# Attention scores as three fp32r products of high and low parts, with both heads' last queries in one block

## What is computed

```python
    scores = scale * np.matmul(q, k.transpose(0, 1, 3, 2))      # scale = 1/8
    scores = np.where(block_i >= block_j, scores, -1000000000.0)  # blocks of 64 positions
    scores = scores - np.max(scores, axis=-1, keepdims=True)
    attn = np.exp(scores)
    attn = attn / (np.sum(attn, axis=-1, keepdims=True) + 1e-09)
    return np.matmul(attn, v).astype(np.float32)
    ...
    h = x @ w_in
    g = np.maximum(h, 0.0) + np.log1p(np.exp(-np.abs(h)))
    return (g @ w_out).astype(np.float32)
```

## Time and profile before

| | us |
|---|---|
| median of three runs | 718.02 |
| lowest, highest | 717.34, 724.31 |
| the profiled execution | 717.23 |
| its span | 715.5 |
| TensorE busy in the span | 680.9 (95%) |
| VectorE, ScalarE, GpSimd busy | 435.8, 404.2, 161.5 |

### The profile page before, as it was taken

The page is one execution under the profiler, slowest core; times in us unless marked ns, Lnnn a source line. Parts: engine busy times, 40 slices in busy tenths (PEclk is TensorE's granted clock), DMA queues, the critical chain, the costliest instruction groups (busy, mean ns, idle before and its releaser), DMA issues.

```text
span 715.5 us, 12988 instructions
## 1 busy us (share of the span) xinstructions
PE 680.9 (95%) x4006; PEld 524.7 (73%) x4006; DVE 435.8 (61%) x1047; ACT 404.2 (56%) x991; POOL 161.5 (23%) x224
## 2 busy tenths in 40 slices
PE   6999999999979999999999999999999999999594
PEld 5565656565568999898888898899889988754342
DVE  5676767676636576667657765776577657824122
ACT  3676667676755566656655666556656655531110
POOL 2867676767620000001000100100020001002011
PEclk9999999999999999999999999999999999999798
DMA  8555755553220000200010011002000100296600
GB/s 192 122 154 134 197 136 156 135 154 103 68 86 1 2 0 1 90 1 10 23 65 1 7 44 44 0 0 66 21 9 3 44 0 3 97 381 197 222 23 17
DMA packets 79616, 53.88 MB, mean 75 GB/s; under 512 B 61208, under 2 KB 64280, under 8 KB 79568
## 3 DMA queue, kind: packets, MB, share of 16 engines
q1 hardware_dynamic: 75872, 50.47, 23.8%
q10 hardware_dynamic: 1920, 1.48, 0.7%
q0 software_dynamic: 1776, 1.33, 0.7%
HBM read 41.31 MB, written 16.28 MB: 80 GB/s over the span
## 4 chain that ended last, share of the span: by engine, by line
PE 62%; DVE 4%; issue 2%; DMA 1%; ACT 1%; ACTq 0%; DVEq 0%; POOL 0%; POOLq 0%
PE hidden L903 9%; PE rows_out L916 9%; PE hidden L905 9%; PE hidden L904 9%; PE rows_out L914 9%; PE rows_out L915 9%; PE hidden L1009 4%; PE rows_out L1023 3%; DMA other_x<-x_sorted 1%; PE turned_y L941 1%; DVE log L1308 1%; DVE g L1309 1%; PE rows_out L1018 1%; PE misc L950 1%; DVE series L1305 1%
## 5 line engine op out<-in xcount | busy, mean ns | idle before, releaser
L903 PE MATMUL hidden<-x_parts,w_in_high 128*128 (+1 forms) x384 | 132.7, 345 | 3.1 <-DVEq L1311 2.9
L1123 ACT ACTIVATE mag<-hidden 128x384 f32<-128x384 f32 x96 | 47.1, 491 | 151.3 <-PE hidden L905 151.1
L905 PE MATMUL hidden<-x_parts,w_in_low 128*128 (+1 forms) x384 | 129.6, 337 | 0.0
L904 PE MATMUL hidden<-x_parts,w_in_high 128*128 (+1 forms) x384 | 129.5, 337 | 0.0
L856 POOL DMA_INDIRECT x_sorted<-y,slot x18 | 20.4, 1136 | 416.6 <-DVE slot L1360 412.9
L916 PE MATMUL rows_out<-w_out_high,g_low 128*128 128x512 f32 x288 | 114.1, 396 | 0.0
L914 PE MATMUL rows_out<-w_out_high,g_high 128*128 128x512 f32 x288 | 113.7, 395 | 0.4 <-DVE g_low L1318 0.4
L915 PE MATMUL rows_out<-w_out_low,g_high 128*128 128x512 f32 x288 | 113.5, 394 | 0.0
L903 PEld LDWEIGHTS hidden<-x_parts,w_in_high 128*128 128x128 f32 x384 | 72.2, 188 | 11.0 <-DVEq L1311 4.1
L444 ACT ACTIVATE probs<-scores,neg_max 128x128 f32<-128x128 f32 (+3 forms) x128 | 67.0, 529 | 20.3 <-DVE neg_max L520 16.5
L266 POOL TENSOR_SCALAR probs<-probs,inverse 128x128 f32<-128x128 f32 (+3 forms) x128 | 65.6, 532 | 51.9 <-DVE inverse L541 51.9
(11 more groups left out here) (169 smaller groups left out, 1065.4 us busy)
## 6 DMA issues: line engine op xcount, KB each, us to landing
whole_w<-in_moe_w_dram SPq DMA_DIRECT2D x12, 1024.0 KB, 10.6
x_heads<-x_pair SPq DMA_DIRECT2D x16, 288.0 KB, 2.1
x_raw<-x_heads SPq DMA_DIRECT2D x6, 768.0 KB, 5.5
out_dram<-y SPq DMA_DIRECT2D x6, 768.0 KB, 4.0
q_nat<-in_q_dram SPq DMA_DIRECT2D x32, 128.0 KB, 2.6
v_nat<-in_v_dram SPq DMA_DIRECT2D x32, 128.0 KB, 2.4
stage<-in_moe_w_in_dram SPq DMA_DIRECT2D x8, 512.0 KB, 3.8
stage<-in_moe_w_out_dram SPq DMA_DIRECT2D x8, 512.0 KB, 4.0
```

The source lines that it names most:

```text
L903: nc.tensor.matmul(o, win["high"][:, k, cols], high, start=(k == 0), stop=False)
L904: nc.tensor.matmul(o, win["high"][:, k, cols], low, start=False, stop=False)
L905: last = nc.tensor.matmul(o, win["low"][:, k, cols], high, start=False, stop=(k == K - 1))
```

## The change

Queries and keys are each kept as a high part, rounded to fp32r, and a low part, the remainder. `qT` becomes `qT["high"]` and `qT["low"]`, `kT` the same. The scores are high x high + high x low + low x high, all in fp32r, which is one pass of the array per product. ScalarE writes the high parts of the full chunks (`round_qk`, two new instructions a step: q between the copies p2a and p2b, k behind the copy p3a), and VectorE writes the low parts in the place of its copies, waiting for ScalarE's. For the ends VectorE does both parts, in six instructions in the place of two.

For block 4 the last 64 queries of both heads stand side by side in `q_last`, 128 columns wide, with zeros where the other head's dimensions are. So one matmul over the whole array serves both heads: six of 288 columns in the place of four (eight records) of 288 columns on quarters. The block's result has the same layout.

For room, q and the tails of q, k and v are loaded into parts of `probsT` that hold no probabilities; the DMAs keep their number, sizes and waits, apart from the addresses.

```diff
+        qT = {h: sb(own, f"qT_{h}", [P, 2, FULL * P], F32R) for h in ("high", "low")}
+        kT = {h: sb(own, f"kT_{h}", [P, 2, S], F32R) for h in ("high", "low")}
+        q_last = {h: sb(own, f"q_last_{h}", [P, 2, P], F32R) for h in ("high", "low")}
...
+        PRODUCTS = (("high", "high"), ("high", "low"), ("low", "high"))
...
                 if i < FULL:
-                    for two in range(2):
-                        d = slice(two * D, two * D + D)
-                        last = nc.tensor.matmul(tile[:, two, :], qT[d, p % 2, P * i:P * i + P],
-                                                kT[d, p % 2, 0:P * (i + 1)], start=True, stop=True)
+                    for a, b in PRODUCTS:
+                        for two in range(2):
+                            d = slice(two * D, two * D + D)
+                            last = nc.tensor.matmul(tile[:, two, :], qT[a][d, p % 2, P * i:P * i + P],
+                                                    kT[b][d, p % 2, 0:P * (i + 1)],
+                                                    start=(a, b) == PRODUCTS[0], stop=(a, b) == PRODUCTS[-1])
                 else:
-                    for n in range(4):
-                        two, half = n % 2, (n // 2 + n) % 2
-                        d = slice(two * D, two * D + D)
-                        last = nc.tensor.matmul(tile[d, half, :], qT[d, p % 2, P * i:S],
-                                                kT[d, p % 2, half * (S // 2):(half + 1) * (S // 2)], start=True, stop=True)
+                    for half in range(2):
+                        for a, b in PRODUCTS:
+                            last = nc.tensor.matmul(tile[:, half, :], q_last[a][:, p % 2, :],
+                                                    kT[b][:, p % 2, half * (S // 2):(half + 1) * (S // 2)],
+                                                    start=(a, b) == PRODUCTS[0], stop=(a, b) == PRODUCTS[-1])
...
+            def round_qk(p, name):
+                at, b = p - 1, p % 2
+                act.wait_ge(s["turned_ready"], turned_count(at, name))
+                if name == "q":
+                    ins = nc.scalar.activation(qT["high"][:, b, 0:P * FULL], bank(at, "q"), ACT.Copy, scale=SCALE)
+                else:
+                    ins = nc.scalar.copy(kT["high"][:, b, 0:P * FULL], bank(at, "k"))
+                ins.then_inc(s["qk_high"], 1)
...
                 if turn:
                     copy_probs(p - 1, "p2a", 2, (0,))
+                if load:
+                    round_qk(p + 1, "q")
+                if turn:
                     copy_probs(p - 1, "p2b", 2, (1,))
...
                 if turn:
                     copy_probs(p - 1, "p3a", 3, (0,))
+                if load:
+                    round_qk(p + 1, "k")
...
                 if name == "q":
-                    ins = nc.vector.tensor_scalar(qT[:, b, 0:P * FULL], bank(at, "q"), SCALE, None, ALU.mult)
+                    dve.wait_ge(s["qk_high"], 2 * p + 1)
+                    ins = nc.vector.scalar_tensor_tensor(qT["low"][:, b, 0:P * FULL], bank(at, "q"), SCALE,
+                                                         qT["high"][:, b, 0:P * FULL], ALU.mult, ALU.subtract)
                 elif name == "k":
-                    ins = nc.vector.tensor_copy(kT[:, b, 0:P * FULL], bank(at, "k"))
+                    dve.wait_ge(s["qk_high"], 2 * p + 2)
+                    ins = nc.vector.tensor_tensor(kT["low"][:, b, 0:P * FULL], bank(at, "k"),
+                                                  kT["high"][:, b, 0:P * FULL], ALU.subtract)
                 else:
-                    nc.vector.tensor_scalar(qT[:, b, P * FULL:S], bank(at, "ends")[:, 0:TAIL], SCALE, None, ALU.mult)
-                    ins = nc.vector.tensor_copy(kT[:, b, P * FULL:S], bank(at, "ends")[:, TAIL:2 * TAIL])
+                    last = slice(P * FULL, S)
+                    q_end, k_end = bank(at, "ends")[:, 0:TAIL], bank(at, "ends")[:, TAIL:2 * TAIL]
+                    own_part = [slice(two * D, two * D + D) for two in range(2)]
+                    for d in own_part:
+                        nc.vector.tensor_scalar(q_last["high"][d, b, d], q_end[d, :], SCALE, None, ALU.mult)\
+                            .then_inc(s["ends_high"], 1)
+                    nc.vector.tensor_copy(kT["high"][:, b, last], k_end).then_inc(s["ends_high"], 1)
+                    for two, d in enumerate(own_part):
+                        dve.wait_ge(s["ends_high"], 3 * p + two + 1)
+                        nc.vector.scalar_tensor_tensor(q_last["low"][d, b, d], q_end[d, :], SCALE, q_last["high"][d, b, d],
+                                                       ALU.mult, ALU.subtract)
+                    dve.wait_ge(s["ends_high"], 3 * p + 3)
+                    ins = nc.vector.tensor_tensor(kT["low"][:, b, last], k_end, kT["high"][:, b, last], ALU.subtract)
                 ins.then_inc(s["copied_by_vector"], 1)
```

More of the change, by code:

```diff
@@ L129, in attention, with v_chunk @@
         probsT = sb(own, "probsT", [P, 2, CH, S])
+        k_nat = sb(own, "k_nat", [P, 2, FULL, 2, D])
+        q_full = [probsT[:, b, FULL, 0:FULL * P].rearrange("p (c a d) -> p c a d", c=FULL, a=2) for b in range(2)]
+        k_full = [k_nat[:, b, :, :, :] for b in range(2)]
+        q_end, k_end, v_end = ([probsT[:, b, c, 0:P].rearrange("p (a d) -> p a d", a=2) for b in range(2)] for c in (1, 2, 3))
+        def v_chunk(p, two, c):
+            return v_nat[:, p % 2, two, c, :] if c < FULL else v_end[p % 2][:, two, :]
         neg_max = sb(own, "neg_max", [P, CH, 2])
@@ L191, in load_qk @@
                     sp.wait_ge(s["turned_ready"], turned_count(p - 3, "ends"))
-                for nat, src, loaded in ((q_nat, qf, q_loaded), (k_nat, kf, k_loaded)) if p > 0 else ((q_nat, qf, q_loaded),):
+                for full, end, src, loaded in ((q_full, q_end, qf, q_loaded), (k_full, k_end, kf, k_loaded))[:2 if p > 0 else 1]:
                     for two in range(2):
-                        sp.dma_start(nat[:, p % 2, 0:FULL, two, :],
+                        sp.dma_start(full[p % 2][:, :, two, :],
                                      src[2 * p + two, 0:FULL * P, :].rearrange("(c p) d -> p c d", p=P))\
                           .then_inc(loaded[p % 2], 16)
-                    sp.dma_start(nat[0:TAIL, p % 2, FULL, :, :],
+                    sp.dma_start(end[p % 2][0:TAIL, :, :],
                                  src[2 * p:2 * p + 2, FULL * P:S, :].rearrange("a p d -> p a d")).then_inc(ends_loaded[p % 2], 16)
@@ L310, in turn_qk @@
                 if name == "ends":
-                    for n, nat in enumerate((q_nat, k_nat)):
+                    for n, end in enumerate((q_end, k_end)):
                         last = nc.tensor.transpose(to[:, n * TAIL:(n + 1) * TAIL],
-                                                   nat[0:TAIL, p % 2, FULL, :, :].rearrange("p a d -> p (a d)"),
+                                                   end[p % 2][0:TAIL, :, :].rearrange("p a d -> p (a d)"),
                                                    ident[0:TAIL, 0:TAIL])
                 else:
-                    nat = q_nat if name == "q" else k_nat
+                    full = q_full if name == "q" else k_full
                     for c in range(FULL):
                         last = nc.tensor.transpose(to[:, c * P:(c + 1) * P],
-                                                   nat[:, p % 2, c, :, :].rearrange("p a d -> p (a d)"), ident[:])
+                                                   full[p % 2][:, c, :, :].rearrange("p a d -> p (a d)"), ident[:])
                 last.then_inc(s["turned_ready"], 1)
@@ L362, in mix_left @@
                     for two in range(2):
-                        last = nc.tensor.matmul(mixed[two * D:two * D + D, 0, P * c:SPLIT], v_nat[:, p % 2, two, c, :],
+                        last = nc.tensor.matmul(mixed[two * D:two * D + D, 0, P * c:SPLIT], v_chunk(p, two, c),
                                                 probsT[:, two, c, P * c:SPLIT], start=(c == 0), stop=(c == 1))
@@ L375, in mix_right @@
                         last = nc.tensor.matmul(mixed[two * D:two * D + D, 1, lo - SPLIT:S - SPLIT],
-                                                v_nat[:, p % 2, two, c, :],
+                                                v_chunk(p, two, c),
                                                 probsT[:, two, c, lo:S], start=(c == 0), stop=(c == CH - 1))
@@ L473, in copy_right @@
                 nc.scalar.copy(x_pair[:, SPLIT:S], mixed[:, 1, 0:S - SPLIT]).then_inc(s["mixed_right_copied"], 1)
+            for name in ("q", "k"):
+                round_qk(0, name)
             for p in range(PAIRS + 2):
-                now, turn = p < PAIRS, 0 < p <= PAIRS
+                now, turn, load = p < PAIRS, 0 < p <= PAIRS, p < PAIRS - 1
                 if p > 1:
@@ L507, in _ @@
             step = Chain(dve, s["sums_step"])
-            nc.vector.memset(v_nat[TAIL:P, :, :, FULL, :], 0.0)
+            for b in range(2):
```

(4 more changed lines are left out.)

16 lines of the change are left out of this document (6 added, 10 removed).

## The result

| | before | after |
|---|---|---|
| median of the timed runs, us | 717.87 (4 runs) | 733.89 (4 runs) |
| lowest, highest | 717.34, 724.31 | 729.79, 737.29 |
| ratio, 95% interval | | 1.0204 [1.0161, 1.0247] |
| the profiled execution, its span | 717.23, 715.5 | 735.79, 734.0 |
| first scores | 8.56 | 9.96 |

Both intervals lie clear of 1 and hold 2%, so the loss is sure and that it is more than 2% is not. The forecast was 722.6 us, with a range of 711.5 to 729.

A forecast was written before the change was run, and what follows sets the result against it. Two balanced loops of about 11.92 us, TensorE's and one through VectorE and GpSimd, were taken to bound the kernel; +4.2 (14 steps), +0.9 (start) and -0.5 (last step) made +4.6, so 722.6 us, range 711.5 to 729.

The forecast's parts named there:

- six at 0.13: VectorE's `ends` copies: six instructions for two at a pitch of 0.13 us, +0.52 us in the loop; step +0.30.
- the stage's end: Last step of the attention stage: loads nothing and keeps the gain of blocks 2 to 4, -0.5 us.
- First scores: Start of the attention stage: first scores move from 8.56 to about 9.70 us, +1.1, or +0.9 after block 3's gain.
- The second loop: Copy of p3b, `ends`, inverse, GpSimd's scalings, p1: sets the changed step at about 12.22 us; chance 0.57.
- p1 waits for GpSimd: Sign of being right: TensorE idles before p1 on GpSimd's scaling, which follows 0.30 us later.
- `ends` for k's low part: Sign of being right: TensorE's `ends` transposes wait for VectorE's low part of k, a stall of 0.32 us.
- The costs of the products: TensorE's score groups: 0.73 us for block 2, 0.90 for block 3; TensorE's work falls by 0.46 to 11.46 per step.
- serialized heads: Rival: the two heads' fp32r products do not run side by side; TensorE's step 13.5 us, total 742; chance 0.10.
- loads that show: Rival: weight loads add 0.4 us in blocks 2 and 3, step 12.6, total 728; chance 0.10, shared with slow short products.
- The rival of GpSimd's port: VectorE's subtractions wait behind GpSimd's split, low q until 107.6; +1.5 us a step, total 743; chance 0.08.
- The rival that TensorE stays the bound: Attention step 11.46 to 11.78 us if the second loop has slack or `ends` is cheaper; 712.0 with 11.46; chance 0.15.
- 0.15 us a step either way: Uncertainty of the likeliest case's step, which with the start gave its own range of 718.5 to 727 us.

The follow-up runs named there:

- e3: Kernel after, with `ends` as four whole-width instructions, second head's last queries not put apart (scores wrong): step 11.88 us against 12.60; 711.25 us, not comparable.
- e11: Kernel after, each of the two half-partition `ends` instructions for q's high part cut in two of 32 columns: step 12.75 us, 740.43 us (one run).
- e6: Kernel after with 19 useless matmuls filling TensorE's gaps at the start and in step 0: 735.56 us, 1.0140 of the kernel before.
- e10: Kernel after, unchanged, measured a second time: 736.18 us, 1.0235 of the kernel before.
- e2: Kernel before with VectorE's early inverse moved ahead of its copy of k: 721.61 us, 1.0029 of the kernel before.
- e12: Kernel after with inverse moved, DMA-built block, filled gaps, k sooner and feed-forward's first load one step later: 714.85 us, 0.9943 of the kernel before.
- e1: Kernel after with VectorE's early inverse moved ahead of its copy of k: 722.28 us, 1.0072 of the kernel before.
- e5: Kernel after with inverse first and q's last queries laid block-diagonally by two DMAs, `ends` four whole-width instructions: 728.00 us, 1.0027 of the kernel before.

## Why the prediction was wrong

The mechanism was right and the sign of its sum too; the size was not, and a second effect was missing.

**The step that failed: "six at 0.13".** The loop, from rows of both kernels:

| part of the loop, us | before | forecast | after |
|---|---|---|---|
| p1 to the copy of p3b | 8.89 | 8.67 | 8.59 |
| copy of p3b to the first of `ends` | 0.61 | 0.61 | 0.61 |
| `ends`, to the inverse | 0.26 | 0.78 | 1.23 |
| inverse to GpSimd | 0.49 | 0.49 | 0.49 |
| GpSimd to p1 | 1.67 | 1.67 | 1.68 |
| step | 11.92 | 12.22 | 12.60 |

The pitch of 0.13 us was read from neighbours of the same 128 partitions and charged for instructions that go from one half to the other and to the whole. Four of the six pitches cross a change of first partition, and there the next instruction waits for the whole length of the one before, 0.22 to 0.26 us instead of 0.13, 0.96 in all instead of 0.52: that is nearly the whole 0.45 us that was missing (e3, e11). The rule of the Trainium skill cited under e11 could have been applied before; with the length of 0.21 us in the earlier trace rows for the four held ones it would have given an estimate of 4 x 0.21 + 2 x 0.13 = 1.10 us for `ends` instead of 0.78, and a step of 12.54. Against it the high part of k came 0.08 us sooner than reckoned. So a step costs +0.68, not +0.30: over 14 steps 9.5 us in the place of 4.2. The pattern of the calculation also stopped one place too early: p1 of the last step waits as well (its `ends` were made in step 14), so the stage's end gave nothing back, +0.38 instead of -0.5.

**What was missing: the clock at the start.** First scores came at 9.96 instead of 9.70, again by the pitch: `ends` takes 1.24 us there too. That TensorE's gaps there grow to 1.15 and 1.44 us, and that the granted clock then falls to 1.2 GHz for 17 us, was in no term: 2.9 us (e6 against e10). That those gaps are the whole cause is not shown (e2, above).

By the profiled attention stage: forecast +4.6, found +13.9. The steps explain 5.3 of the 9.3 us between, the clock 2.9, and the last step and the start's pitch 1.1. Between the forecast 722.6 and the median 733.9 lie 11.3 us, so 2 more stay open. The pitch alone would have made 728, still in the range; it took the clock as well to leave it.

**What held.** The second loop, invisible in TensorE's busy share, sets the step; p1 waits for GpSimd and `ends` for k's low part. The costs of the products held to 0.01 us, those of 64 rows included: heads side by side, no weight load visible in groups of 384 and 512 columns. The rivals of serialized heads and of loads that show fell; the row tells against the sentence in "TensorE: Matmul & The Clock Gate" of the Trainium skill (Part 3, The mechanism) that a weight load overlaps only a matmul in other rows, as it did in the stream of full-array products. The rival of GpSimd's port fell too: q's low part took 0.69 us at 115.44, inside GpSimd's split of 114.39 to 116.76, and not 1.21 as in the earlier trace rows. What "SBUF — State Buffer" of the Trainium skill (Who interferes with whom) says of an operation with at most one SBUF input, that it does not contend, agrees with this row. The rival that TensorE stays the bound was false for this kernel, but its price was nearly right: with the second loop shortened (e12) the same products run in 11.60.

**The range.** It ended at 729 because the bounds that were worked out were nearly all on TensorE's side. The deciding loop had 0.15 us a step either way, from no row, and its new term, six times 0.13, a single value and no upper bound, although no row showed an instruction on one half of the partitions next to one on the other.

## What to carry to other kernels

- Two loops in balance share one busy row. Before costing an edit, find the waits whose sum is small but whose count is about that of the steps, add up that loop from rows, and charge the edit to each loop by itself.
- A pitch between instructions is a fact about that pair of neighbours, their first partitions included. Where the loop that decides gets a new kind of neighbour, that term needs its upper bound first; and it pays to let the DMA lay data out so that the engine works on whole width.
- Look at the granted clock wherever an edit lengthens a wait of TensorE at the start, and try the cheap order changes (a small instruction ahead of a long one) before judging a change by its time. Here one such move gave back most of the loss (e1), and with the layout by the DMA, the filled gaps, k sooner and the later load +2% became -0.6% (e12).

## What the runs showed of the hardware

- VectorE: neighbours of 32 or 64 columns that begin at the same partition start 0.10 to 0.14 us apart, those that begin at another one 0.20 to 0.26.
- TensorE: two fp32r products on 64 rows each, of different heads, take together 0.11 us at 128 columns, 0.12 at 256, 0.18 at 384 and 0.24 at 512. One of the whole array takes 0.13 at 288.
- TensorE: the two transposes of `ends` take 0.17 us to the next group with both on the whole array (e12), 0.24 with both on 64 rows (after), 0.43 with one of each (e5).
- The clock: two gaps of 1.15 and 1.44 us within the first 10 us, and the granted clock was at 1.2 GHz for the next 17 us; with the gaps filled it was not (e6). It also fell for 3.4 us in e2, whose gaps were nearly those of the kernel before, which kept 2.4 GHz.
